# A Fourier-mix and two-layer FFN kernel: zero products ahead of the eleventh tile, first matrices and first read back issued by ScalarE, mixing weights converted in halves, inverse loads one step sooner, two P1 copies on ScalarE

## The reference

```
X  = rfft(x, axis=1)                      # 3008 = 47 * 64 points
Yr = Xr @ w_r - Xi @ w_i + b_r;  Yi = Xr @ w_i + Xi @ w_r + b_i
Y  = sign(Y) * max(abs(Y) - 0.01, 0)      # real and imaginary part apart
x  = irfft(Y, n=3008, axis=1)             # 6016 tokens of 256
h  = x @ w_in;  g = max(h, 0) + alpha * min(h, 0);  x = g @ w_out    # 256 -> 2048 -> 256
h  = x @ w_in2; g = 0 if h <= -1, h if h >= 1, else (h + 1)^2 / 4;  out = g @ w_out2
```

## Time and profile before

| | before |
|---|---|
| median of the runs | 1193.59 us |
| profiled execution, its own time | 1193.44 us |
| its span, first to last instruction | 1191.6 us |
| mean granted TensorE clock | 0.996 |
| TensorE matmul busy | 1173.8 us (98%) |
| VectorE busy | 886.9 us (74%) |
| ScalarE busy | 850.6 us (71%) |
| GpSimd busy | 693.0 us (58%) |

### The profile page before, as it was taken

How to read it: one execution, slowest core, us unless ns; L and a number is a source line. 1 busy time by engine, 2 the same in 40 slices (tenths; PEclk the granted TensorE clock), 3 DMA queues, 4 the chain that set the end, 5 groups by cost and what they waited for, 6 DMA issues and landing times.

```text
span 1191.6 us, 21169 instructions
## 1 busy us (share of the span) xinstructions
PE 1173.8 (98%) x6948; PEld 1135.4 (95%) x6948; DVE 886.9 (74%) x1686; ACT 850.6 (71%) x1874; POOL 693.0 (58%) x724
## 2 busy tenths in 40 slices
PE   8999999999999999999999999999999999999997
PEld 3899889999999999999999999999999999999997
DVE  3787777767777777777777787778777777878765
ACT  2435557767777777777777688888888787878775
POOL 3006646666575766667557566666657575757553
PEclk9999999999999999999999999999999999999999
DMA  8777620211112201202005500101010101010001
GB/s 309 246 252 238 192 63 1 94 40 54 41 58 63 67 28 41 87 35 67 19 1 177 194 19 2 26 1 27 1 28 1 27 2 25 2 17 11 13 15 27
DMA packets 64126, 77.76 MB, mean 65 GB/s; under 512 B 31216, under 2 KB 43632, under 8 KB 64016
## 3 DMA queue, kind: packets, MB, share of 16 engines
q1 hardware_dynamic: 60532, 69.92, 19.1%
q10 hardware_dynamic: 3484, 6.48, 1.6%
HBM read 46.10 MB, written 30.28 MB: 64 GB/s over the span
## 4 chain that ended last, share of the span: by engine, by line
PE 92%; POOL 3%; DMA 1%; ACT 1%; issue 1%; DVE 1%; SPq 0%; POOLq 0%; DVEq 0%; ACTq 0%
PE bank L1159 79%; PE bank L1126 5%; PE bank L1145 2%; POOL g_lo L514 2%; PE bank L1100 2%; PE bank L1136 2%; PE bank L1111 2%; DMA ut<-inverse_scratch 1%; DMA x_sb<-x 1%; POOL prep_raw L540 0%; POOL xc_lo L490 0%; DMA slots_scratch<-a_sb 0%; PE bank L1084 0%; ACT g_hi L757 0%; POOL prep_raw L525 0%
## 5 line engine op out<-in xcount | busy, mean ns | idle before, releaser
L514 POOL TENSOR_TENSOR g_lo<-g_sb,g_hi 128x376 fp32r<-128x376 f32 x510 | 506.3, 1004 | 368.3 <-ACT g_hi L757 367.7
L1159 PE MATMUL bank<-g_hi,w_out_hi 128*128 128x376 f32 x1024 | 344.9, 337 | 1.6 <-POOL g_lo L514 1.3
L1159 PE MATMUL bank<-g_lo,w_out_hi 128*128 128x376 f32 x1024 | 341.9, 334 | 0.0
L1159 PE MATMUL bank<-g_hi,w_out_lo 128*128 128x376 f32 x1024 | 341.7, 334 | 0.0
L1159 PE MATMUL bank<-xc_hi,w_in_hi 128*128 128x376 f32 x896 | 302.0, 337 | 1.4 <-DVE g_sb L960 0.9
L1159 PE MATMUL bank<-xc_hi,w_in_lo 128*128 128x376 f32 x896 | 300.3, 335 | 0.0
L1159 PE MATMUL bank<-xc_lo,w_in_hi 128*128 128x376 f32 x896 | 298.5, 333 | 0.0
L757 ACT ACTIVATE g_hi<-g_sb 128x376 fp32r<-128x376 f32 x512 | 261.1, 510 | 43.4 <-DVE g_sb L960 27.7
L1159 PEld LDWEIGHTS bank<-g_hi,w_out_hi 128*128 128x128 f32 x1024 | 192.4, 188 | 9.8 <-POOL g_lo L514 8.5
L1159 PEld LDWEIGHTS bank<-g_hi,w_out_lo 128*128 128x128 f32 x1024 | 192.4, 188 | 0.0
L1159 PEld LDWEIGHTS bank<-g_lo,w_out_hi 128*128 128x128 f32 x1024 | 192.4, 188 | 0.0
(11 more groups left out here) (82 smaller groups left out, 1537.2 us busy)
## 6 DMA issues: line engine op xcount, KB each, us to landing
gc<-group_consts SPq DMA_DIRECT2D x24, 256.0 KB, 4.3
zt<-slots_scratch SPq DMA_DIRECT2D x24, 256.0 KB, 4.1
inverse_scratch<-v_sb SPq DMA_DIRECT2D x24, 256.0 KB, 2.7
ut<-inverse_scratch SPq DMA_DIRECT2D x16, 384.0 KB, 5.0
slots_scratch<-a_sb ACTq DMA_DIRECT2D x15, 384.0 KB, 4.1
x_sb<-x SPq DMA_DIRECT2D x16, 256.0 KB, 4.0
prep_raw<-wpack SPq DMA_DIRECT2D x16, 256.0 KB, 2.6
out<-yt SPq DMA_DIRECT2D x120, 32.0 KB, 1.6
```

What stands on the lines that cost most here:

```text
L514: pool.tensor_tensor(g_lo[kind][:, :], g_sb[n % 3][:, :], g_hi[kind][:, :].bitcast(f32), ALU.subtract)\
L1159: done = pe.matmul(out_ap, w, g, start=first and n == 0, stop=last_one and n == 2, skip_group_check=unchecked)
```

## The change

Six things are edited. (1) TensorE gets two products of zeros (WAIT_PRODUCTS) ahead of the eleventh tile, t = 10. (2) The load of the first constants `gc` (pair 0) is issued by ScalarE after its store of the eighth tile, and the read back of the first `zt` by ScalarE after its copy of the tenth tile; both leave SyncE's queue, and SyncE's wait for the stores of batch 0 stands behind the loads of the mixing weights, of the thirteenth tile and of the bias. (3) The high and low part of the mixing weights are made in two halves of 512 columns. (4) The first two loads of `ut` are issued in pass 17 of SyncE's loop and not in pass 18. (5) The copies of P1 of groups 0 and 1 are ScalarE's. (6) In group 0 VectorE does the second part of C11 ahead of u3.

```diff
--- before.py
+++ after.py
@@ -25,6 +25,7 @@
 VECTOR_FILLS = 6
 HALF_COLS = TILE_COLS // 2
 WARM_PRODUCTS = 2
+WAIT_PRODUCTS = 2
 FF = 2048
 FC = FF // P
 LAM = 0.01
@@ -60,6 +61,7 @@
 PREP_FROM, PREP_EVERY = 4, 3
 TAKE_FROM = LAYER_GROUPS - FP
 GC_SLOTS = 4
+P1_BY_SCALAR = 2
 LOW_ON_VECTOR = [(ALL_GROUPS - 1, C21), (ALL_GROUPS - 1, C12)]
 
 
@@ -365,12 +367,10 @@
                          a_tile(t)[:, HALF_COLS:]).then_inc(a_stored[0], 16)
             load_x(TILES_PER_BATCH + 2)
             load_x(TILES_PER_BATCH + 3)
-            load_matrices(0)
-            sp.wait_ge(a_stored[0], 16 * (TILES_PER_BATCH + 1))
-            load_values(0)
             sp.dma_start(wm_raw[:, :], wmix).then_inc(wm_in, 16)
             load_x(FIRST_TILES)
             sp.dma_start(bias_sb[:, :], bias).then_inc(bias_in, 16)
+            sp.wait_ge(a_stored[0], 16 * (TILES_PER_BATCH + 1))
             for p in range(1, SLOTS):
                 load_values(p)
                 load_matrices(p)
@@ -389,7 +389,7 @@
                 for n in range(FP):
                     if p == 9 + 3 * n // 2:
                         load_weights(n)
-                if p == 18:
+                if p == 17:
                     for i in range(SLOTS):
                         sp.wait_ge(v_stored[i], 16 * (PAIRS // 2 // SLOTS))
                     load_u(0)
@@ -598,8 +598,15 @@
                 copy_a(t, a_bank[(2 * t) % 4])
                 if t < TILES_PER_BATCH:
                     store_a(t)
+                if t == TILES_PER_BATCH - 1:
+                    act.dma_start(gc[0][:, :], group_consts[0, :, :]).then_inc(gc_in[0], 16)
+                if t == TILES_PER_BATCH + 1:
+                    act.wait_ge(a_stored[0], 16 * (TILES_PER_BATCH + 1))
+                    act.dma_start(zt[0][:, :, :], az_pairs[0, :, :, :]).then_inc(zt_in[0], 16)
             act.wait_ge(wm_in, 16)
-            act.activation(wm_hi[:, :], wm_raw[:, :], ACT.Copy).then_inc(wm_hi_ready, 1)
+            for part in range(2):
+                cols = slice(part * 2 * D, (part + 1) * 2 * D)
+                act.activation(wm_hi[:, cols], wm_raw[:, cols], ACT.Copy).then_inc(wm_hi_ready, 1)
 
             def split_xt(s):
                 slot = s % SLOTS
@@ -698,8 +705,19 @@
                 if at == 3:
                     kept_hi(q, B22, t + 1, 1)
 
+            def take_p1(g):
+                act.wait_ge(p1_done, g + 1)
+                if g:
+                    act.wait_ge(h_ready[C22], g)
+                else:
+                    act.wait_ge(win_lo_ready, FP)
+                    act.wait_ge(wout_lo_ready, FP)
+                act.activation(partial[:, :], c11_bank[:, 0:N], ACT.Copy).then_inc(p1_left, 1)
+
             for s in range(STEPS):
                 split_xt(s)
+                if s == STEPS - 1:
+                    take_p1(0)
                 if s in LATE_TILES:
                     copy_a(LATE_TILES[s], a_bank[0])
                 if s >= 2:
@@ -798,6 +816,8 @@
                 if g < ALL_GROUPS:
                     high(g, C11)
                     first_part(g, C22)
+                    if g + 1 < P1_BY_SCALAR:
+                        take_p1(g + 1)
                 if at == 0:
                     keep(q - 1, 0)
                 if g < ALL_GROUPS:
@@ -829,9 +849,11 @@
 
             for t in range(FIRST_TILES):
                 copy_a(t, a_bank[(2 * t + 1) % 4])
-            dve.wait_ge(wm_hi_ready, 1)
-            dve.tensor_tensor(wm_lo[:, :], wm_raw[:, :], wm_hi[:, :].bitcast(f32), ALU.subtract)\
-               .then_inc(wm_lo_ready, 1)
+            for part in range(2):
+                cols = slice(part * 2 * D, (part + 1) * 2 * D)
+                dve.wait_ge(wm_hi_ready, part + 1)
+                dve.tensor_tensor(wm_lo[:, cols], wm_raw[:, cols], wm_hi[:, cols].bitcast(f32), ALU.subtract)\
+                   .then_inc(wm_lo_ready, 1)
 
             def split_xt(s):
                 slot = s % SLOTS
@@ -885,21 +907,10 @@
                 dve.wait_ge(t_lo_ready, t_lo_count(q, T1))
                 dve.tensor_tensor(r[1][:, :], side_bank[:, 0:N], r[0][:, :], ALU.subtract).then_inc(t_made, 1)
 
-            def take_p1(g):
-                dve.wait_ge(p1_done, g + 1)
-                if g:
-                    dve.wait_ge(h_ready[C22], g)
-                else:
-                    dve.wait_ge(win_lo_ready, FP)
-                    dve.wait_ge(wout_lo_ready, FP)
-                dve.tensor_copy(partial[:, :], c11_bank[:, 0:N]).then_inc(p1_left, 1)
-
             for s in range(STEPS):
                 split_xt(s)
                 if s in LATE_TILES:
                     copy_a(LATE_TILES[s], a_bank[1])
-                if s == STEPS - 1:
-                    take_p1(0)
                 if s:
                     threshold(s - 1)
                 if s == 5:
@@ -921,6 +932,13 @@
                     side_t4(0)
 
             def make_u2(g):
+                if g >= P1_BY_SCALAR:
+                    dve.wait_ge(p1_done, g + 1)
+                    dve.wait_ge(h_ready[C22], g)
+                    dve.tensor_copy(partial[:, :], c11_bank[:, 0:N]).then_inc(p1_left, 1)
+                elif g == 0:
+                    dve.wait_ge(win_lo_ready, FP)
+                    dve.wait_ge(wout_lo_ready, FP)
                 dve.wait_ge(p6_done, g + 1)
                 dve.wait_ge(p1_left, g + 1)
                 if g:
@@ -1040,8 +1058,6 @@
 
             for g in range(ALL_GROUPS + 1):
                 q, at = divmod(g, FP)
-                if 1 < g < ALL_GROUPS:
-                    take_p1(g)
                 if g < ALL_GROUPS:
                     make_u2(g)
                 second_part(g - 1, C12)
@@ -1055,7 +1071,10 @@
                 if g == 0:
                     threshold(STEPS - 1)
                     dve.wait_ge(neg_ready, 1)
-                if g < ALL_GROUPS:
+                if g == 0:
+                    second_part(g, C11)
+                    make_u3(g)
+                elif g < ALL_GROUPS:
                     make_u3(g)
                     second_part(g, C11)
                 tokens_second(q + 1, at)
@@ -1067,8 +1086,6 @@
                     leave(q - 1, 0, 0)
                 if g < ALL_GROUPS:
                     make_c12(g)
-                    if g == 0:
-                        take_p1(1)
                     second_part(g, C21)
                 if at == 0:
                     leave(q - 1, 0, 1)
@@ -1115,7 +1132,7 @@
 
             def mix(s):
                 if s == 0:
-                    pe.wait_ge(wm_lo_ready, 1)
+                    pe.wait_ge(wm_lo_ready, 2)
                 pe.wait_ge(xt_lo_ready, s + 1)
                 if s:
                     pe.wait_ge(y_sum_ready, s)
@@ -1254,6 +1271,8 @@
                 last.then_inc(out_done, 1)
 
             for t in range(FIRST_TILES):
+                if t == TILES_PER_BATCH + 2:
+                    idle_products(WAIT_PRODUCTS)
                 real47(t, [a_bank[(2 * t + part) % 4] for part in range(2)])
             for s in range(STEPS):
                 forward(s)
```

## The result

The changed kernel took 1191.59 us in the median of 15 runs (1190.21 to 1193.41), the kernel before 1194.23 us in 15 runs beside it (1192.89 to 1197.28). The ratio is 0.9977, 95% interval 0.9969 to 0.9984: 2.7 us less (1.9 to 3.7), where 3.5 were forecast. 1190.1 us was the time forecast, and 1191.59 is within the range, 0.2 us from its upper end. The ratio is on the faster side of the 0.2% that the prediction took as its line, but its interval holds that line. The profiled execution took 1192.74 us, 1.2 above that median; its span is 1190.9 us, 0.7 less than that of before, and one has to say stage by stage which part of the difference is the change.

The account below looks back on a forecast made before the run. TensorE's waits (input tiles, `ut`, the P1 copy, `g_lo`) were taken to bound the kernel. Savings 1.2 + 1.3 + 1.0 = 3.5 us gave 1190.1 us against the median of 1193.59; the 8-in-10 range was 1188.9 to 1191.8.

Parts of the forecast that it names:

- the 0.2% that the prediction took as its line: Whole kernel: a measurement can tell 0.2%, 2.4 us, from no change; "faster" means below 1191.2 us.
- Part 2: `ut` issued a pass sooner: TensorE's whole wait for it goes, 1.3 us, from 1.2 to 1.4.
- rival E: Pair 18 onward: the extra 768 KB never gets worked off, pairs 18 to 23 come late, 1194.9 us; chance 0.04.
- Part 3: Group 0: P1(1) comes sooner as its 0.88 us wait for `g_sb` goes; 1.0 us, from 0.3 to 1.4.
- Rival C: Group 0: ScalarE's chain bounds, the copy delays C21 by 0.5 us, sum 2.9, 1190.7 us; chance 0.12.
- the prediction's own sign of being wrong: Group 0: ScalarE's first part of C21 starts at once behind its copy of P1, and C21 was ready before.
- Part 1: Start: thirteenth tile issued and landing sooner (1.0 us), weights in halves (0.2); 1.2 us, from 0 to 1.5.
- Rival B: Start: thirteenth tile bound by volume, lands near 32.3; start gains 0 to 0.3, sum 2.3 to 2.6, 1191.1 us; chance 0.14.
- The clock and the zeros: Start: zeros fill 1.8 of the 2.15 us wait, preventing a clock fall; without them the 1.0 us is lost.
- the delay by `gc`: Start: `gc` ahead of the eleventh tile may delay it by 0.8 us, to 26.2 us.
- The halves of the weights: Ahead of `mix(0)`: conversion takes 1.8 in place of 2.3 us, which removes a 0.2 us loss.
- Its lower end: Range that holds 8 in 10: 1188.9 us, every term near its upper end, 4.3 to 4.7 saved.

Follow-up runs that it names:

- e2_ut_only: The kernel before with only the first two loads of `ut` moved from pass 18 to pass 17; 1192.38 us, ratio 0.9987 to before.
- e3_p1_only: The kernel before with only ScalarE's copies of P1 and C11's second part ahead of u3; 1193.08 us, ratio 0.9992 to before.
- e1_start_only: The kernel before with only the start's changes (zeros, load order, weights in halves); 1193.89 us, ratio 1.0005 to before.
- e9_wait_first: The changed kernel with SyncE's wait for the stores of batch 0 moved back ahead of the mixing weights' load; 1191.85 us, ratio 0.9980 to before.
- e4_no_zeros: The changed kernel without the two products of zeros ahead of the eleventh tile; 1191.66 us, ratio 0.9975 to before.
- e10_extra_load: The changed kernel with one more 256 KB load ahead of the mixing weights on SyncE's queue; 1192.40 us, ratio 0.9990 to before.
- e12: The changed kernel with the load order of before and no zeros, keeping the weights in halves and the ut and P1 changes; 1191.21 us, ratio 0.9977 to before.
- e13_ten_first: e12 with ten tiles in the first stage in place of twelve, two moved to the second; 1194.17 us, ratio 0.9994 to before.
- e15_ten_zeros: e13_ten_first with four products of zeros between the tenth tile and `forward(0)`; 1192.12 us, ratio 0.9985 to before.

## Why the prediction was right, and where it was not

**Part 2, `ut` sooner: right.** 1.3 us forecast, 1.6 by `e2_ut_only` (0.6 to 2.6), 1.5 by the traces. The pair behind it did not wait, and rival E, the queue that never catches up, did not happen.

**Part 3, P1 and C11: right, in its working too.** 1.0 us forecast; 1.1 by the trace, 1.0 by `e3_p1_only` with zero just inside its interval. P1(1) follows `inverse(47)`, the wait for the copy turned into a longer one for `g_lo` (1.25 us) as stated. Rival C came close: ScalarE's first part of C21 started 0.02 us behind its copy, the first half of the prediction's own sign of being wrong. The second half did not come: C21 was ready at 163.16 us, 0.01 before the copy ended, so the copy delayed nothing, and its room was used up.

**Part 1, the start: wrong.** 1.2 us forecast, no gain measured (-1.7 to +0.5 by `e1_start_only`). The step that failed is the one that made of the sooner issue of the thirteenth tile a sooner `mix(0)`: "With `gc` and `zt` gone from this queue, the weights take the place of `gc`, so weights and tile are issued 1.2 us sooner", and then 1.0 of them taken as gain. The sooner issue did come, though not in the profiled execution: the weights were issued at 24.0 to 25.5 us in the five traces with that order, 24.6 on average, and at 24.9 to 26.2, 25.4 on average, in the five with the order of before. It did not become a sooner `mix(0)`. I followed the transfer that landed last in the trace of before and did not work out the landing of the one that it overtakes. `zt` is just as needed, it has more work behind it (`forward` and then the tile's products, where the tile has its own alone: 2.9 us and 2.2), and it went from 3.9 to 6.0 us between issue and landing (five traces) to 6.3 to 8.0 (five traces with the changed order). Rival B had the right result by nearly the right cause: 2.3 to 2.6 us was its saving, and 1191.1 us its time, 0.5 below the median measured. It is also what the Trainium skill says in "DMA: Bandwidth & Descriptors", "Issuing engines are not separate DMA queues": the transfers of the two issuers interleave on the same engines. The traces agree: `zt` landed after 3.9 to 6.0 us when it stood ahead of the weights in one queue, and after 7.0 when issued at the same moment as they from another (`e9_wait_first`), while that other queue moved 1.63 MB. I had cited the rule, and given the case 0.14.

**The clock and the zeros: a term that could not count.** I argued that without the zeros the 1.0 us would be lost. `e4_no_zeros` loses nothing. Nor did the zeros hold the clock every time: in the changed kernel's trace 1.62 us idle after them were enough for it to fall, in `e10_extra_load` 1.69 us were not. Of the six traces with zeros there it fell in three, of the six with twelve tiles and no zeros in four. I had put the eleventh tile at 26.2 us from one trace. Its products began at 26.3 to 27.7 in the seven traces with `gc` ahead of it, 27.1 on average, and at 25.5 to 27.1, 26.1 on average, in the five without. So the delay by `gc`, 0.8 us in the prediction, was about right, and the starting point was an early one.

**The halves of the weights: right by the traces, without use in the new order.** The 0.2 us of this term is below what the times can tell; the traces show 0.25 where the tile lands last (`e12`). In the changed order `mix(0)` did not wait for the weights.

So the total came within its range because two terms of three were right and the range had been drawn to hold the failure of one; had one more failed, it would not have held. Its lower end is also not what the terms give: their upper ends are 1.5, 1.4 and 1.4 us, 4.3 in all, which is 1189.3 us, not 1188.9.

## What to carry to other kernels

When a transfer is moved ahead in a stretch where the DMA engines are full, work out the landing of every transfer that it passes, and how much work stands behind each: an order can only choose who is last, and the last should be the one with the least behind it. Putting an urgent load on a second engine's queue takes its place in line away from it. A wait that ends in a transfer hides a slow clock; ask what stands between the last landing and the next stage before paying for a warm one, and do not take the idle time in one trace as the budget.

## What the runs showed of the hardware that was not expected

- The start scatters from execution to execution by more than its edits are worth: the first read back was issued between 24.48 and 25.75 us in the five traces of the table with the load order of before, on the same program up to there.
- The granted clock was 1.00 through tiles 10 and 11 in the trace of `e3_p1_only` after 2.27 us of waiting, and at half in that of before after 2.15 us, with the same instructions. In `e1_start_only` it fell after 1.51 us of waiting for `ut`. How long a wait is does not by itself tell whether the clock falls.
- Read back right behind its store and with little else under way, 256 KB landed in 2.6 us (`e13_ten_first`, `e15_ten_zeros`); in the other traces the same load took 3.9 to 8.0 us.
